# Half of the attention thresholds on VectorE instead of GpSimd, and a ring of 8 kept tiles instead of 10

## The reference

```
scores = q @ k.T / sqrt(64)
thresh = max(scores, axis=-1) - tau            # tau = 0.02
scores = where(scores >= thresh, scores, -1e9)
attn   = exp(scores - max(scores)); attn /= sum(attn) + 1e-9
x      = attn @ v                              # to [2304 tokens, 512]
```

## Time and profile before

| | before |
|---|---|
| median of 3 (range) | 882.21 us (880.66 to 882.29) |
| the profiled execution | 882.21 us, span 880.5 us |
| mean granted TensorE clock | 0.994 |
| PE busy | 861.0 us, 98% |
| DVE busy | 628.8 us, 71% |
| ACT busy | 565.8 us, 64% |
| POOL busy | 343.4 us, 39% |

### The profile page before, as it was taken

How to read it: one execution, slowest core, us unless ns; L and a number is a source line. 1 busy time by engine, 2 the same in 40 slices (tenths; PEclk the granted TensorE clock), 3 DMA queues, 4 the chain that set the end, 5 groups by cost and what they waited for, 6 DMA issues and landing times.

```text
span 880.5 us, 16881 instructions
## 1 busy us (share of the span) xinstructions
PE 861.0 (98%) x6248; PEld 718.6 (82%) x6248; DVE 628.8 (71%) x1214; ACT 565.8 (64%) x1040; POOL 343.4 (39%) x497
## 2 busy tenths in 40 slices
PE   7999999999999999999999999999999999999998
PEld 4666666666667889889899999999999999999996
DVE  6899999999946552624557678768768768858865
ACT  4788997888876442523365667667666666667664
POOL 4665878666636401202111233223322332332232
PEclk9799999999999999999999999999999999999999
DMA  6723422343001000000022400000000000000000
GB/s 168 205 48 83 109 72 66 83 109 124 3 1 49 25 0 1 1 1 1 1 85 60 167 1 1 36 1 1 36 1 1 36 1 1 36 0 0 36 0 36
DMA packets 30393, 37.15 MB, mean 42 GB/s; under 512 B 4720, under 2 KB 18544, under 8 KB 30320
## 3 DMA queue, kind: packets, MB, share of 16 engines
q1 hardware_dynamic: 29920, 35.90, 14.6%
q10 hardware_dynamic: 400, 0.30, 0.1%
HBM read 31.46 MB, written 4.72 MB: 41 GB/s over the span
## 4 chain that ended last, share of the span: by engine, by line
PE 54%; issue 25%; POOL 12%; DVE 7%; ACT 2%; POOLq 0%; DVEq 0%; ACTq 0%
PE h_ps L1034 12%; PE y_ps L1170 11%; POOL w_lo L528 9%; PE m_ps L1146 8%; PE f_ps L1235 7%; PE s_ps L1066 7%; PE o_ps L1106 4%; DVE ntop L838 4%; DVE kept L848 2%; ACT expd L581 2%; PE t_ps L1082 1%; PE lt_ps L1182 1%; POOL w_lo L442 1%; POOL thresh L458 1%; PE s_ps L1061 1%
## 5 line engine op out<-in xcount | busy, mean ns | idle before, releaser
L1146 PE MATMUL m_ps<-y_hi,w 128*128 128x384 f32 x768 | 211.8, 337 | 0.0
L528 POOL TENSOR_TENSOR w_lo<-w_rest,w_hi 128x512 fp32r<-128x512 f32 x84 | 109.5, 1304 | 253.9 <-ACT w_hi L701 253.7
L1146 PEld LDWEIGHTS m_ps<-y_hi,w 128*128 128x128 f32 x768 | 140.3, 188 | 3.9
L581 ACT ACTIVATE expd<-s_ps,ntop 128x576 f32<-128x576 f32 x144 | 104.8, 740 | 47.3 <-DVE ntop L838 47.3
L1146 PE MATMUL m_ps<-y_lo,w 128*128 128x384 f32 x384 | 129.0, 336 | 0.0
L701 ACT CAST w_hi<-w_rest 128x512 fp32r<-128x512 f32 x84 | 52.2, 622 | 109.0 <-PE f_ps L1235 104.7
L838 DVE TENSOR_REDUCE ntop<-s_ps 128x1 f32<-128x576 f32 x144 | 106.1, 756 | 18.8 <-PE s_ps L1066 13.0
L848 DVE SCALAR_TENSOR_TENSOR kept<-s_ps,thresh,expd 128x576 f32<-128x576 f32 x144 | 112.3, 816 | 4.4 <-POOL thresh L458 1.0
L1235 PE MATMUL f_ps<-w_hi,g_hi 128*128 128x512 f32 x288 | 113.4, 394 | 0.7 <-POOL w_lo L528 0.7
L1235 PE MATMUL f_ps<-w_hi,g_lo 128*128 128x512 f32 x288 | 113.8, 395 | 0.0
L1235 PE MATMUL f_ps<-w_lo,g_hi 128*128 128x512 f32 x288 | 112.8, 392 | 0.0
(11 more groups left out here) (88 smaller groups left out, 1682.5 us busy)
## 6 DMA issues: line engine op xcount, KB each, us to landing
q_sb<-q_t SPq DMA_DIRECT2D x28, 288.0 KB, 5.0
v_sb<-v_main SPq DMA_DIRECT2D x16, 256.0 KB, 3.1
stage<-w_in SPq DMA_DIRECT2D x16, 256.0 KB, 2.7
out<-o_sb SPq DMA_DIRECT2D x5, 768.0 KB, 3.6
w_rest<-w_out SPq DMA_DIRECT2D x7, 512.0 KB, 5.4
k_sb<-k_t SPq DMA_DIRECT2D x21, 144.0 KB, 4.7
stage<-w_in SPq DMA_DIRECT2D x4, 512.0 KB, 8.3
stage<-w_out SPq DMA_DIRECT2D x4, 512.0 KB, 6.4
```

Source lines behind the costliest of these rows:

```text
L528: nc.gpsimd.tensor_tensor(w4[1][n % 2], w4_rows(n % F2, 1)[:, 0, :], f32(w4[0][n % 2]), ALU.subtract).then_inc(w4lo_made, 1)
L581: nc.scalar.activation(expd[:, tile % 2, :].rearrange("p (a b) -> p a b", a=2), s_ps[tile % 2][:, :, 0:HALF], ACT.Exp, bias=ntop[:, tile % ...
L1146: last = nc.tensor.matmul(m_ps[n % 4][:, 0:GC], w[n % F2][:, k, :], y[odd][:, k, :], start=(k == 0 and m == 0), stop=(k == C - 1 and m == 2))
```

## The change

The threshold of every odd tile (b) is made by DVE, in a new instruction right behind `maximum(b)`; POOL makes only those of even tiles (a). There are two semaphores, `thresh_a` and `thresh_b`, in place of `thresh_made`. The DVE instruction waits for the semaphore of DVE's own `maximum(b)`. RING goes from 10 to 8, and PAD1 grows by the 1152 words that this frees.

```
-RING = 10
+RING = 8
-PAD1, PAD2 = 4480, 865
-SCORE_WORDS = 13056
+PAD1, PAD2 = 5632, 865
+        SCORE_WORDS = PAD1 + 4 * QCOLS + 4 * SEQ
-        ATT_WORDS = (PAD1 + 4 * QCOLS + 4 * SEQ + 4 * (KT + 1) * 2 * DH + ...
+        ATT_WORDS = (SCORE_WORDS + 4 * (KT + 1) * 2 * DH + ...
-        thresh_made = sem("thresh_made")
+        thresh_a, thresh_b = sem("thresh_a"), sem("thresh_b")

 POOL
-            def make_threshold(tile):
-                pool.wait_ge(top_made, tile + 1)
-                col = slice(tile % 4, tile % 4 + 1)
+            def make_threshold_a(u):
+                pool.wait_ge(top_made, 2 * u + 1)
+                col = slice(2 * u % 4, 2 * u % 4 + 1)
                 nc.gpsimd.tensor_scalar(thresh[:, col], ntop[:, col], -1.0, tau_sb[:, 0:1], ALU.mult, ALU.subtract
-                                        ).then_inc(thresh_made, 1)
+                                        ).then_inc(thresh_a, 1)
...
                 if u < DOUBLES:
-                    make_threshold(2 * u)
-                    make_threshold(2 * u + 1)
+                    make_threshold_a(u)

 DVE
+            def make_threshold_b(u):
+                col = slice((2 * u + 1) % 4, (2 * u + 1) % 4 + 1)
+                dve.wait_ge(top_made, 2 * u + 2)
+                nc.vector.tensor_scalar(thresh[:, col], ntop[:, col], -1.0, tau_sb[:, 0:1], ALU.mult, ALU.subtract
+                                        ).then_inc(thresh_b, 1)
             def keep(tile):
                 dve.wait_ge(exp_made, tile + 1)
-                dve.wait_ge(thresh_made, tile + 1)
+                dve.wait_ge((thresh_a, thresh_b)[tile % 2], tile // 2 + 1)
                 wait(dve, left_made, (tile - RING) // 2 + 1)
...
                 if u < DOUBLES:
                     maximum(b)
+                    make_threshold_b(u)
                 for group in complete(u - 1):
                     if group != GROUPS - 2:
                         invert(group)
```

More of the change, by code:

```diff
@@ L133, in build @@
         phase.close()
-        ATT_WORDS = (PAD1 + 4 * QCOLS + 4 * SEQ + 4 * (KT + 1) * 2 * DH + (2 + RING) * SEQ + (KT + 1) * PCOLS * P
+        SCORE_WORDS = PAD1 + 4 * QCOLS + 4 * SEQ
+        ATT_WORDS = (SCORE_WORDS + 4 * (KT + 1) * 2 * DH + (2 + RING) * SEQ + (KT + 1) * PCOLS * P
                      + 2 * 4 + 4 * SIX + PAD2)
```

## The result

The changed kernel takes 887.92 us (median of 5, 885.83 to 888.94) against 882.18 us (median of 5, 880.66 to 882.29): a ratio of 1.0064 with a 95% interval of 1.0047 to 1.0082. It is slower by 5.7 us, where the forecast was 3.1 us.

What follows compares the result with a forecast made beforehand. The prediction took the attention stage's loop of keep(a), next scores, maximum and exponential as the bound. It added 2.7 us (steady doubles) and 0.4 us (first doubles) to 882.21 us, giving 885.3 us, range 882.9 to 889.2 us.

Steps and rivals of the forecast that it cites:

- likely case: Whole kernel: the prediction's own forecast of 883.9 to 887 us, given a chance of 0.57.
- slower rival: Attention stage: short covers fail and a stopped queue adds 0.07 to each of two instructions; 887 to 892 us, chance 0.14.
- What sets the pace: Attention stage: the exponential, not DVE's queue, sets keep(a), at 1.56 us after M, the start of a double's first maximum.
- the chain's 1% for POOL's thresholds: Attention stage: these 8.8 us look like a prize, but keeps left DVE idle for a threshold only 1.0 us in all.
- The ring at 0: Kept tiles: 8 slots instead of 10 cost 0, since PE does the freeing transposes ahead of the same double's scores.
- The wait for its own maximum, 0.13: DVE's new threshold instruction: waiting for its predecessor's result starts it 0.13 us later than the next instruction starts now.
- It then holds the queue for 0.07: DVE's new threshold instruction: it occupies DVE's queue for 0.07 us, read from an instruction in the second stage.
- remainder 2: Doubles with u mod 3 = 2: keep(a) at M + 1.69 instead of 1.56, 0.13 later in 21 doubles, 2.7 us.
- Remainder 1: Doubles with u mod 3 = 1: cost 0, the exponential hides the threshold with only 0.03 us to spare.
- Remainder 0: Doubles with u mod 3 = 0: keep(a) comes 0.12 us later, covered by PE's slack of about 0.2 us.
- Sum: Whole kernel: 2.7 us from the steady part and 0.4 us from the first doubles, 3.1 us slower.
- First doubles: Start of attention stage, u = 4 and 5: nothing hides the instruction, 0.20 us each, 0.4 us for both.

Runs made afterwards that it cites:

- e4: Changed kernel in which POOL still also computes the threshold of b, into a spare column nobody reads; 886.40 us.
- e1: Kernel before the change with only the ring of 8 kept tiles and the larger pad; 880.41 us, ratio 1.0004.
- e3: Changed kernel whose DVE threshold instruction reads the maximum of a, so it does not wait (wrong thresholds for odd tiles); 880.36 us, ratio 1.0001 to the kernel before.
- e2: Changed kernel whose DVE threshold instruction takes the constant 0.02 instead of tau from memory; 887.47 us.
- e6: Changed kernel whose DVE threshold instruction takes the constant 0.02 and reads the maximum of a, so it does not wait (wrong thresholds); 879.80 us.
- e5: Changed kernel with DVE's threshold instruction behind the reciprocal instead of in front of it; 882.58 us, 0.19% slower than the kernel before.
- e8: Kernel before without threshold instructions: keep compares and reads the exponential, and PE's next scores wait for the exponential instead of keep; 897.99 us.

## Why the prediction was right, and which terms were off

The measured 887.92 us lies inside the stated 882.9 to 889.2 us, and the direction, the path and the price of the wait were right. But the likely case, 883.9 to 887, missed it, and the cost was nearly twice the forecast. The terms that were off, below, all made the forecast too small; none of them cancelled another. The range held because its upper end took in most of the slower rival, and with some luck of the clock: the forecast started from 882.2 us, an execution at a mean granted clock of 0.994, and at that clock the changed kernel took 888.9 us, 0.3 below the end of the range.

- *What sets the pace.* Right. The exponential set `keep(a)` before (1.567 in all three kinds), and the chain's 1% for POOL's thresholds was no prize: e4 shows that POOL's share changes nothing.
- *The ring at 0.* Shown by e1 in time and distances.
- *The wait for its own maximum, 0.13.* Right in mechanism and size: 0.12 (e3, M + 1.41 against M + 1.53).
- *"It then holds the queue for 0.07."* Mis-sized: 0.13 in the changed kernel. I had taken it from an instruction with constants. e2 and e6 show that it is 0.06 to 0.08 with constants and 0.12 to 0.13 with tau from memory (e3 and after), but also that behind a stop the keep would have come only 0.005 earlier with the constant. With this term right, remainder 2 gives 1.50 + 0.04 + 0.13 + 0.08 = 1.75, measured 1.745: 0.178 late instead of 0.13.
- *Remainder 1: cost 0, "hidden by the exponential with only 0.03 to spare".* This is the cover that failed: 0.086 per period, 24 x 0.086 = 2.1 us. Both reasons had been named, the short cover of the exponential and that of the scores of b behind a late `keep(b)`, and both gave way: the first once the hold was 0.13 (0.02 of the 0.086), the second because its cover was 0.12 (0.17 less 0.06, see e5) and `keep(b)` of the double before came 0.19 late (0.06 of it).
- *Remainder 0: PE covers it.* Right: 0.196 late, and 0.179 of it came back in the hand-over to PE (1.859 to 1.680). The slack that I put at 0.2 was just used up. PE's weight loads for the scores waited 6.0 us longer for `kept` in all (54.5 instead of 48.5 us from 20 to 260 us), where 3 was forecast.
- *Sum.* 0.178 + 0.086 + 0.196, less 0.179 + 0.007 + 0.005 in the hand-overs, is 0.269 per period against 0.13 forecast; the forecast's likely case ended at 887.0, and the result, 887.9, lies in the slower rival's part of the range. That rival was right in one point, that a stopped queue gets going slowly, but not in the size: it adds 0.07 to each of the next two instructions, which makes 0.29 from threshold to keep, and 0.27 late; measured were 0.21 and 0.178. And it put remainder 1 at 0.04, where 0.086 was lost.
- *First doubles.* Forecast to the start of double 12: 0.4 us, and 2 x 0.13 for u = 8 and 11, 0.66 in all. Measured was 0.54, but with the clock of 18 to 34 us at 0.68 before and 0.89 after. e2, whose period differs from the changed kernel's by 0.015, ran this stretch at 0.68 too: double 12 started at 50.49, 0.96 us later than before. So this term was too small as well: two periods lie in doubles 6 to 11, and at 0.25 each they alone make 0.5.

## What to carry over

An instruction that waits for the one right before it on its own engine costs far more than its row: here 72 rows of 0.21 us cost about 0.5 us without the wait (e3) and more than 6 us with it. Part of that is not in the instruction at all: the waits of the instructions behind it are worked off only after the stop. If such an instruction must be there, put independent small work between it and its source; that took back 0.15 of the 0.27 us per period (e5). And where several covers of 0.03 to 0.15 us lie around a loop, test the forecast with the term at twice its size: which covers give way then is the better estimate of the risk than the term itself.

## Hardware behaviour that I had not expected

- The granted TensorE clock in the first 34 us differs between executions and accounts for much of their scatter. As a mean from 18 to 34 us it was 0.68 in the profiles before and of e1, 0.89 after, 1.00 in e5 and e6 (1.0 being 2.4 GHz and 0.5 its lower level of 1.2 GHz). Double 12 started at 49.53 us before and at 47.00 us in e6, whose period is the same: 2.5 us. Of the 46 executions of the kernel before beside the experiments, 28 took 879.2 to 880.1 us at a mean granted clock of 0.998 to 1.0, and 15 took 882.3 to 882.75 at 0.994. In the profile before the clock was 0.5 from 20.7 to 30.9 us; in that of the changed kernel from 29.0 to 32.4; in e6 it did not fall there. PE had been busy for only 0.29 of the 2 us from 18 to 20 us, before the fall; in e6 it was 0.41. What decides it, the runs do not show.
- Behind a stop of DVE's queue, the keep follows the threshold after 0.21 us, with the reciprocal between them, with a threshold row of 0.15 as with one of 0.21 (e2 and after). With no reciprocal between (remainder 1) it is 0.11 and 0.13. A wait instruction whose semaphores are long up still took 0.05 us there, and the keep came 0.05 behind its end; in a running queue (e3, e6) the same wait ended 0.36 to 0.41 us before the keep.
- With both inputs in SBUF a keep took 0.82 us while POOL was quiet, and 1.23 us on average, at most 1.82, when it started while POOL worked on SBUF (e8).
